# Attention feeding two mixture-of-experts layers: k's leading parts cast on ScalarE one head further ahead, a finished batch's routing and squares spread anew over eight heads

## The chip, the cores and the metric

One core of one Trainium2 chip. The metric is the device time of one execution in microseconds, taken as the median of several runs; lower is better.

## What is computed

Three stages, one feeding the next. q, k, v are 4 batches x 8 heads x 576 rows x 64 columns; f is a forget gate per row. The two expert layers have 8 experts each, 512 -> 1024 -> 512, and every token goes to its best expert alone.

```python
scores = scale * q @ k.T + cum[:, None] - cum[None, :]      # cum = cumsum(log f), causal mask
attn = softmax(scores); x = (attn @ v), heads side by side   # 2304 tokens x 512
# layer 1: expert = argmax(cosine of x and expert_emb), gate = its softmax probability (with tau)
# layer 2: expert = argmax(x @ w_gate), gate = its softmax probability
out = gate * relu(x @ w1[expert]) @ w2[expert]
```

All matrix products are kept near fp32: an operand is split into a leading part (a cast to fp32r, a float32 form that TensorE takes) and the rest, and the products of leading x leading, rest x leading and leading x rest are summed.

## The kernel before, in words

Every engine has its own instruction stream, written out by hand in the order in which it runs; the streams meet only through semaphores. There is no planner. A wait at the head of a stream holds back all that stands behind it on that engine.

**Attention** takes the first 270 us or so: a loop over 32 heads (h = 8 b + hh, batch b, place hh) on every engine. In head h TensorE does the transposed scores of head h (`by_key`, five blocks, L407) and, between them, the plain scores of head h+1 (`by_query`, L395), whose row minima serve as the softmax shift. It then does `weighted` (probabilities times v, L426), turns the finished output of head h-1 back (`back`, L437), brings the minima of head h+1 into one row (`minima_row`, L419), and ends with the last three `weighted` blocks. `by_key(h+1, 0)` waits for `row_ready`.

- SyncE (loop at L336) issues the loads. In pass h it loads q and k of head h+2, each twice, once for either half of the partitions (`load_qk`, L289: q, k, q, k), then the cumulative rows, then, after `pv_done >= h` (the weighted sums of head h-1), v of head h+2. In even passes from 16 on it loads a chunk of expert weights (L358). In passes 6, 10, 14, ... it stores half a batch of finished rows (`store_rows`, L361 to L363).
- ScalarE (L711): `keep_ot(h-1)` copies the output sums out of PSUM, `exps(h, 0..4)` take the exponentials, `leading_q(h+2)` (L661) casts q after the third of them, and `row_in(h+1)` (L675) at the end brings the row of minima into the operand and raises `row_ready`. Between `exps(h, 4)` and `row_in` stand, in batches 1 to 3, the squares of the rows of the finished batch (`g_square`, L685, five per batch), the exponential of its logits (`route_exp`, L691), and, in the eight odd heads from 17 on (SPLIT_AT), the cast of a weight chunk (`split_hi`, L700).
- VectorE (L1127): `leading_k(h+2)` (L823, the cast of k, 128 x 576), one `routing_step` of the finished batch (L1104), the masked minima of head h+1 (`mins`, L861, five blocks) with `rest_k(h+2)` (L837) between, `rest_q(h+2)` (L830), `norm(h-1)` (L903), which waits for `back`, and `split_lo` (L1086) in the SPLIT_AT heads.
- GpSimd (L1344): `copy_k(h+2)` (L1289) copies the cast k for a second operand and stands first in the pass, so behind `leading_k(h+2)`; then `clear(h, 0..4)` (L1294) zero the masked triangle of each exponential block, with `copy_q(h+2)` between. `norms` (L1329) and `scatter` (L1336, table entries of a finished batch by indirect DMA) end the passes named in the diff.

k of head h is held raw in one of two buffers (`k_raw`), its cast in one of three (`kA`). `weighted(h, 0)` waits for `clear(h, 0)`. TensorE waits for all five `mins` before `back` and `minima_row`, and for `rank_read` at hh = 3, `first_read` at hh = 0 and `vals_done` at the end of hh = 7.

**The expert layers** (about 290 to 903 us) are two loops over experts and their tiles of 128 tokens. The change does not touch them.

Of the kernel before, what the change touches and what calls it, by code (L numbers as in the profile page):

```python
# [21 lines left out]
def attention_moe_moe(nc, q_t, k_t, v_p, f, emb_t, tau, w1a, w2a, wg, w1b, w2b, out):  # L22
    B, H, D, S = q_t.shape
    E, DM, FF = w1a.shape
    HEADS = B * H
    TOK = B * S
    NRT = TOK // P
    QT = (S + P - 1) // P
# [26 lines left out]
    with ExitStack() as ctx:  # L55
# [3 lines left out]
        def sem(name):  # L59
            return ctx.enter_context(nc.semaphore(name))  # L60

        def sems(name, n):
            return [sem(f"{name}{i}") for i in range(n)]
# [65 lines left out]
        def asb(name, shape, dt=F32):  # L129
            return attention.enter_context(nc.sbuf_tensor(name, shape, dt))  # L130
# [3 lines left out]
        k_raw = [asb(f"k_raw{a}", [2 * D, S]) for a in range(2)]  # L134
# [3 lines left out]
        kA = [asb(f"kA{a}", [2 * D, SP_], F32R) for a in range(3)]  # L138
# [71 lines left out]
        q_in, k_in, c_in, v_in = sems("q_in", 2), sems("k_in", 2), sems("c_in", 3), sems("v_in", 3)  # L210
        q_hi, k_hi, q_cp, k_cp, q_lo, k_lo = (sem(n) for n in ("q_hi", "k_hi", "q_cp", "k_cp", "q_lo", "k_lo"))
        s_done, t_done = sems("s_done", QT), sems("t_done", QT)
# [444 lines left out]
        def _(act):  # L657
# [3 lines left out]
            def leading_q(h):  # L661

                act.wait_ge(q_in[h % 2], (h // 2 + 1) * 32)
                if h >= 3:
                    act.wait_ge(t_done[QT - 1], h - 2)
                act.mul(qA[h % 3][:], q_raw[h % 2][:], SCALE).then_inc(q_hi, 1)

            def exps(h, t):

                act.wait_ge(t_done[t], h + 1)  # L670
                M = P if t < FT else LR
                act.activation(probT[0:M, PT_AT[t]:PT_AT[t] + S - t * P], ps[0:M, T_AT[t]:T_AT[t] + S - t * P], ACT.Exp,  # L672
                               scale=-1.0).then_inc(exps_done, 1)
# [11 lines left out]
            def g_square(b, t, width=DM):  # L685
                sq = act.activation(squares[:, t, 0:width], o_rows[b % 2][:, t, 0:width], ACT.Square,
                                    accum_out=ssq[:, b * QT + t:b * QT + t + 1])
                if t == QT - 1:
                    sq.then_inc(ssq_done, 1)
# [21 lines left out]
            for h in range(HEADS):  # L711
                b, hh = h // H, h % H
                if h > 0:
                    keep_ot(h - 1)
                exps(h, 0)
                exps(h, 1)
                exps(h, 2)
                if h + 2 < HEADS:
                    leading_q(h + 2)
                exps(h, 3)  # L720
                exps(h, 4)
                if b > 0 and hh == 1:
                    act.wait_ge(norm_done, b * H)
                    g_square(b - 1, 0)
                    g_square(b - 1, 1)
                if b > 0 and hh == 2:
                    g_square(b - 1, 2)
                    g_square(b - 1, 3)
                if b > 0 and hh == 3:
                    g_square(b - 1, 4)  # L730
                if b > 0 and hh == 5:
                    route_exp(b, b - 1)
                if h in SPLIT_AT:
                    split_hi(0, SPLIT_AT.index(h), 1)
                if h + 1 < HEADS:
                    row_in(h + 1)
# [62 lines left out]
        def _(dve):  # L799
# [23 lines left out]
            def leading_k(h):  # L823

                dve.wait_ge(k_in[h % 2], (h // 2 + 1) * 32)
                if h >= 3:
                    dve.wait_ge(t_done[QT - 1], h - 2)
                dve.tensor_copy(kA[h % 3][:, 0:S], k_raw[h % 2][:]).then_inc(k_hi, 1)  # L828

            def rest_q(h):  # L830
# [171 lines left out]
            def place_batch(b):  # L1002

                lo = b * QT
                link(dve.tensor_reduce(rank_f[:, lo:lo + QT], pos[:, lo:lo + QT, :], AX.X, ALU.add),
                     dve.tensor_reduce(ohs[:], oh[:, lo:lo + QT, :].rearrange("p g e -> p e g"), AX.X, ALU.add))
                link(dve.tensor_copy(rank_i[:, lo:lo + QT], rank_f[:, lo:lo + QT]),
                     dve.tensor_tensor(scum[0][:], scum[0][:], ohs[:], ALU.add))
                dve.sem_inc(sum_done, 1)

            def enter_batch(b):

                lo = b * QT
                ent = entry0[:, lo:lo + QT, :]
                link(dve.tensor_scalar(rtile_i[:, lo:lo + QT], rank_i[:, lo:lo + QT], 7, None, ALU.arith_shift_right))
                link(dve.scalar_tensor_tensor(out=part_f[:, lo:lo + QT], in0=rtile_i[:, lo:lo + QT], scalar=1.0 - P * SPP,
                                              in1=region[:, lo:lo + QT], op0=ALU.mult, op1=ALU.add))
                dve.scalar_tensor_tensor(out=ent[:, :, 3], in0=rank_f[:, lo:lo + QT], scalar=float(SPP),
                                         in1=part_f[:, lo:lo + QT], op0=ALU.mult, op1=ALU.add)

            def key_batch(b):

                lo = b * QT
                link(dve.scalar_tensor_tensor(out=key[:], in0=first_i[:, lo:lo + QT], scalar=2.0 * P, in1=rank_f[:, lo:lo + QT],
                                              op0=ALU.mult, op1=ALU.add))
# [78 lines left out]
            def routing_step(b, hh):  # L1104

                if hh == 0 and b > 1:
                    add_firsts(b - 2)
                if hh == 1:
                    largest_batch(b - 1)
                if hh == 2:  # L1110
                    choose_batch(b - 1)
                if hh == 3:
                    read_ranks(b - 1)
                    place_batch(b - 1)
                if hh == 4:
                    key_batch(b - 1)
                    hot_batch(0)
                    hot_batch(1)
                if hh == 5:
                    enter_batch(b - 1)  # L1120
                    scale_batch(b - 1)
                if hh == 6:
                    gate_batch(b - 1)
                if hh == 7:
                    parts_batch(b - 1)

            for h in range(HEADS):  # L1127
                b, hh = h // H, h % H
                n, m = h + 1, h + 2
                if m < HEADS:  # L1130
                    leading_k(m)
                if b > 0:
                    routing_step(b, hh)
                if n < HEADS:
                    mins(n, 4)
                    mins(n, 3)
                if m < HEADS:
                    rest_k(m)
                if n < HEADS:
                    mins(n, 2)  # L1140
                    mins(n, 1)
                    mins(n, 0)
                if m < HEADS:
                    rest_q(m)
                if h == 0:
                    embedding_rows()
                    token_columns()
                else:
                    norm(h - 1)
                if h in SPLIT_AT:  # L1150
                    split_lo(0, SPLIT_AT.index(h), 1)
# [110 lines left out]
        def _(pool):  # L1262
# [73 lines left out]
            def scatter(b, tiles):  # L1336

                pool.wait_ge(ent_done[0], b + 1)
                for t in tiles:
                    pool.indirect_dma_start(out=tab[0], out_offset=bass.IndirectOffsetOnAxis(  # L1340
                        ap=entry0[:, b * QT + t, 3:4], axis=0), in_=entry0[:, b * QT + t, :], in_offset=None,
                        bounds_check=E * TOK - 1, oob_is_err=False).then_inc(g_ent_out, 16)

            for h in range(HEADS):  # L1344
                b, hh = h // H, h % H
                if h + 2 < HEADS:
                    copy_k(h + 2)
                clear(h, 0)
                clear(h, 1)
                clear(h, 2)  # L1350
                if h + 2 < HEADS:
                    copy_q(h + 2)
                clear(h, 3)
                clear(h, 4)
                if b > 0 and hh == 4:
                    norms(b - 1)
                if b == 1 and hh == 6:
                    pool.wait_ge(s_init, 64)
                if b > 0 and hh >= 6:
                    scatter(b - 1, range(hh - 6, hh - 5))  # L1360
                if b > 1 and hh < QT - 2:
                    scatter(b - 2, range(hh + 2, hh + 3))
            scatter(B - 2, range(2, QT))
            norms(B - 1)
            chain = Counter(pool, "pool_chain", pchain[0])

# [127 lines left out]
```

## Time and profile before

| what | us |
|---|---|
| median of 3 runs | 910.94 |
| the three runs | 904.73, 910.94, 911.35 |
| the profiled execution, its own time | 905.14 |
| its span, first to last instruction | 903.6 |

| engine | busy us | share of the span |
|---|---|---|
| TensorE matmuls (PE) | 862.4 | 95% |
| TensorE weight loads (PEld) | 709.3 | 79% |
| VectorE (DVE) | 575.3 | 64% |
| ScalarE (ACT) | 403.8 | 45% |
| GpSimd (POOL) | 293.9 | 33% |

The span is the time between the first and the last instruction; the execution's own time has 1.5 us around it. Busy shares are averages over stages with different limits. The ends of matmuls are modelled, so TensorE may show as busy while it waits briefly. Numbers in the prediction are from the one profiled execution. SPq is SyncE's queue.

### The profile page before, as it was taken

To read this page: it belongs to the slowest core of one execution; us is meant where nothing else is said; L and a number is where in the kernel's file an instruction comes from. 1 tells how busy PE (TensorE), PEld (TensorE's weight loads), DVE (VectorE), ACT (ScalarE), POOL (GpSimd) and SP (SyncE) were. 2 spreads that over 40 slices of the span, in tenths; PEclk is the share of its full clock that TensorE was granted. 3 is DMA by queue.
4 is the path that set the end of the run, shared out by engine and by line. 5 is a ranking of instruction groups with operands and counts; after the bars stand their busy time and mean duration, and the time that the engine had idled before them with its cause. 6 is when DMAs were issued, how large, how long until landed. Compare 5 with 4: busy or idle time off the path is not lost.

```text
span 903.6 us, 16352 instructions
## 1 busy us (share of the span) xinstructions
PE 862.4 (95%) x5025; PEld 709.3 (79%) x5026; DVE 575.3 (64%) x1723; ACT 403.8 (45%) x708; POOL 293.9 (33%) x459
## 2 busy tenths in 40 slices
PE   6999999999997899999999999969999999999995
PEld 5788777777776788888888888858888888888884
DVE  7777888888876576757487767536652264425643
ACT  2455645646652553535265535205551254324541
POOL 7344455345435422233133222222122121122120
PEclk7999999999999999999999999989999999999998
DMA  4334444544522854334265544306652162516100
GB/s 133 95 103 128 128 123 131 152 141 126 169 63 72 296 172 170 124 129 160 98 206 172 169 156 136 113 26 227 217 187 95 35 226 69 189 41 223 46 26 23
DMA packets 59244, 119.63 MB, mean 132 GB/s; under 512 B 11934, under 2 KB 20638, under 8 KB 59204
## 3 DMA queue, kind: packets, MB, share of 16 engines
q1 hardware_dynamic: 49620, 96.93, 33.2%
q0 software_dynamic: 9440, 22.18, 7.5%
q8 instruction: 19, 0.31, 0.1%
q14 instruction: 21, 0.17, 0.1%
q10 hardware_dynamic: 144, 0.04, 0.0%
HBM read 104.13 MB, written 17.99 MB: 135 GB/s over the span
## 4 chain that ended last, share of the span: by engine, by line
PE 80%; DVE 11%; DMA 3%; issue 3%; SPq 1%; POOL 1%; ACT 0%; POOLq 0%; DVEq 0%; ACTq 0%
PE ps L636 27%; PE ps L607 26%; PE ps L445 8%; PE ps L432 5%; PE ps L440 4%; DVE ps L868 3%; PE ps L450 2%; PE ps L403 2%; PE ps L415 2%; PE ps L416 1%; PE ps L404 1%; DVE kA L840 1%; DMA k_raw<-in_k 1%; DVE kA L828 1%; DVE hot L1029 1%
## 5 line engine op out<-in xcount | busy, mean ns | idle before, releaser
L1089 DVE TENSOR_TENSOR wlo<-stage,whi 128x1024 fp32r<-128x1024 f32 x136 | 160.0, 1221 | 31.8 <-ACT whi L703 30.3
L703 ACT CAST whi<-stage 128x1024 fp32r<-128x1024 f32 x136 | 133.6, 1057 | 0.0
L768 ACT ACTIVATE h_s<-ps 128x512 f32<-128x512 f32 x44 | 26.3, 598 | 219.9 <-PE ps L607 219.9
L432 PE MATMUL ps<-probT,v_s 128*65 128x448 f32 (+4 forms) x384 | 103.3, 391 | 3.5 <-POOL probT L1299 3.4
L636 PE MATMUL ps<-whi,hT_hi 128*128 128x512 f32 x352 | 99.5, 404 | 0.0
L636 PE MATMUL ps<-whi,hT_lo 128*128 128x512 f32 x352 | 99.1, 403 | 0.0
L607 PE MATMUL ps<-whi,xT_hi 128*128 128x512 f32 x352 | 94.9, 392 | 3.0 <-DVE xT_lo L1195 3.0
L607 PE MATMUL ps<-whi,xT_lo 128*128 128x512 f32 x352 | 95.2, 392 | 0.0
L636 PE MATMUL ps<-wlo,hT_hi 128*128 128x512 f32 x352 | 95.0, 392 | 0.0
L607 PE MATMUL ps<-wlo,xT_hi 128*128 128x512 f32 x352 | 94.9, 392 | 0.0
L868 DVE CUSTOM_DVE_ANT_0 ps<-ps,maskf 128x576 f32<-128x576 f32 (+4 forms) x160 | 75.3, 510 | 20.6 <-PE ps L404 19.2
L672 ACT ACTIVATE probT<-ps 128x576 f32<-128x576 f32 (+4 forms) x160 | 66.2, 435 | 41.8 <-PE ps L416 38.1
L607 PEld LDWEIGHTS ps<-whi,xT_hi 128*128 128x128 f32 x352 | 65.7, 188 | 18.2 <-ACT xT_hi L759 3.5
L636 PEld LDWEIGHTS ps<-wlo,hT_hi 128*128 128x128 f32 x352 | 66.2, 188 | 14.7
L607 PEld LDWEIGHTS ps<-wlo,xT_hi 128*128 128x128 f32 x352 | 66.1, 188 | 14.7
L607 PEld LDWEIGHTS ps<-whi,xT_lo 128*128 128x128 f32 x352 | 66.2, 188 | 14.2
L1227 DVE TENSOR_TENSOR hT_lo<-ps,hT_hi 128x512 fp32r<-128x512 f32 x44 | 30.4, 690 | 71.4 <-ACT hT_hi L775 71.2
L636 PEld LDWEIGHTS ps<-whi,hT_lo 128*128 128x128 f32 x352 | 63.0, 189 | 11.2
L636 PEld LDWEIGHTS ps<-whi,hT_hi 128*128 128x128 f32 x352 | 62.8, 188 | 11.1
L415 PE MATMUL ps<-qB,kB 97*128 97x288 f32 (+2 forms) x192 | 69.5, 371 | 0.3 <-ACT probT L672 0.3
L1371 POOL COPY ent_next<-ent_tab 128x4 int32 (+1 forms) x45 | 8.6, 192 | 182.8 <-DVE ent_mid L1196 181.5
L1243 DVE COPY y_idx<-ent_cur 128x1 int32<-128x1 int32 x44 | 6.7, 152 | 94.2 <-PE ps L636 94.2
(223 smaller groups left out, 1626.6 us busy)
## 6 DMA issues: line engine op xcount, KB each, us to landing
stage<-in_moe_w SPq DMA_DIRECT2D x128, 512.0 KB, 4.3
q_raw<-in_q SPq DMA_DIRECT2D x64, 144.0 KB, 3.0
k_raw<-in_k SPq DMA_DIRECT2D x64, 144.0 KB, 3.1
v_s<-in_v SPq DMA_DIRECT2D x32, 162.5 KB, 2.3
x<-o_rows SPq DMA_DIRECT2D x8, 512.0 KB, 3.9
kB<-cum_hl SPq DMA_DIRECT2D x64, 2.2 KB, 1.7
table<-entry POOLq DMA_INDIRECT x44, 2.5
table<-tinit SPq DMA_DIRECT2D x2, 288.0 KB
```

Source lines behind the costliest of these rows:

```text
L415: pe.matmul(o, kB[a][0:ROW + 1, k0:k0 + P], qB[a][0:ROW + 1, lo:hi], start=True, stop=False)
L432: mm = pe.matmul(ps[0:D + 1, OT_AT + lo:OT_AT + hi], v_s[h % 3][:, t, :], probT[:, col:col + hi - lo], start=(t == 0), stop=(t == QT - 1 o ...
L440: mm = pe.matmul(back_ps[:, t, :], o_t[:, t * P:(t + 1) * P], i_emb[:, h % H, :], start=True, stop=True)
L445: mm = pe.transpose(bank[:, c * P:(c + 1) * P], src[:, c * P:(c + 1) * P], ident[:])
L607: mm = pe.matmul(h_ps[hf], x[:, c * P:(c + 1) * P], w1_sl(w[b], c, hf * 512, 512), start=(wi == 0 and c == 0), stop=(wi == 2 and c == DC - 1))
L636: mm = pe.matmul(y_ps, h[:, kk * P:(kk + 1) * P], w2_sl(w[b], kk), start=(hf == 0 and wi == 0 and kk == 0), stop=(hf == 1 and wi == 2 and ...
L672: act.activation(probT[0:M, PT_AT[t]:PT_AT[t] + S - t * P], ps[0:M, T_AT[t]:T_AT[t] + S - t * P], ACT.Exp, scale=-1.0).then_inc(exps_done, 1)
L703: act.copy(whi[b][:, c, :], stage[:, c, :]).then_inc(w_hi[c], 1)
L768: act.activation(h_s[:, 0:512], h_ps[0], ACT.Relu).then_inc(h_relu[0], 1)
L868: dve.tensor_tensor_reduce(out=tile, in0=tile, in1=maskf[0:M, at:at + q1], scale=1.0, scalar=LARGE, op0=ALU.add, op1=ALU.min, accum_out=sm ...
L1089: dve.tensor_tensor(wlo[b][:, c, :], stage[:, c, :], whi[b][:, c, :].bitcast(F32), ALU.subtract).then_inc(w_lo[c], 1)
L1227: dve.tensor_tensor(hT_lo[:, 0:512], hT_ps[0], hT_hi[:, 0:512].bitcast(F32), ALU.subtract).then_inc(h_lo[0], 1)
```

## The change

- `leading_k` for heads 2 and up moves from VectorE to ScalarE. ScalarE does it for head h+3 after `exps(h, 4)`, ahead of the squares, the weight cast and `row_in`; in head 0 also for head 2, between `leading_q(2)` and `exps(0, 3)`. VectorE keeps heads 0 and 1. The new one waits for `k_in`, both halves of k of head h+3.
- The squares of a finished batch are spread as 1, 2, 1, 1 over hh = 1 to 4 (before 2, 2, 1 over hh = 1 to 3); its `route_exp` moves from hh = 5 to 6.
- On VectorE: `key_batch` from hh = 4 to 3, `enter_batch` from 5 to 4, the two `hot_batch` from 4 to 5, `scale_batch` from 5 to 6, `gate_batch` from 6 to 7; `parts_batch` stays in 7.
- On GpSimd the scatters of a batch move by one head: tile 0 in hh = 7, tiles 1 to 4 in hh = 0 to 3 of the batch after, and for batch 2 its tiles 1 to 4 after the loop (before: tiles 0 and 1 in hh = 6 and 7, tiles 2 to 4 in hh = 0 to 2, or after the loop).

```diff
+            def leading_k(h):
+
+                act.wait_ge(k_hi, h)
+                act.wait_ge(k_in[h % 2], (h // 2 + 1) * 32)
+                act.copy(kA[h % 3][:, 0:S], k_raw[h % 2][:]).then_inc(k_hi, 1)
...
                 if h + 2 < HEADS:
                     leading_q(h + 2)
+                if h == 0:
+                    leading_k(2)
                 exps(h, 3)
                 exps(h, 4)
+                if h + 3 < HEADS:
+                    leading_k(h + 3)
                 if b > 0 and hh == 1:
                     act.wait_ge(norm_done, b * H)
                     g_square(b - 1, 0)
+                if b > 0 and hh == 2:
                     g_square(b - 1, 1)
-                if b > 0 and hh == 2:
                     g_square(b - 1, 2)
+                if b > 0 and hh == 3:
                     g_square(b - 1, 3)
-                if b > 0 and hh == 3:
+                if b > 0 and hh == 4:
                     g_square(b - 1, 4)
-                if b > 0 and hh == 5:
+                if b > 0 and hh == 6:
                     route_exp(b, b - 1)
...
             def leading_k(h):
 
                 dve.wait_ge(k_in[h % 2], (h // 2 + 1) * 32)
-                if h >= 3:
-                    dve.wait_ge(t_done[QT - 1], h - 2)
                 dve.tensor_copy(kA[h % 3][:, 0:S], k_raw[h % 2][:]).then_inc(k_hi, 1)
...
                 if hh == 3:
                     read_ranks(b - 1)
                     place_batch(b - 1)
+                    key_batch(b - 1)
                 if hh == 4:
-                    key_batch(b - 1)
+                    enter_batch(b - 1)
+                if hh == 5:
                     hot_batch(0)
                     hot_batch(1)
-                if hh == 5:
-                    enter_batch(b - 1)
+                if hh == 6:
                     scale_batch(b - 1)
-                if hh == 6:
+                if hh == 7:
                     gate_batch(b - 1)
-                if hh == 7:
                     parts_batch(b - 1)
...
-                if m < HEADS:
-                    leading_k(m)
...
-                if b == 1 and hh == 6:
+                if b == 1 and hh == 7:
                     pool.wait_ge(s_init, 64)
-                if b > 0 and hh >= 6:
-                    scatter(b - 1, range(hh - 6, hh - 5))
-                if b > 1 and hh < QT - 2:
-                    scatter(b - 2, range(hh + 2, hh + 3))
-            scatter(B - 2, range(2, QT))
+                if b > 0 and hh == 7:
+                    scatter(b - 1, range(1))
+                if b > 1 and hh < QT - 1:
+                    scatter(b - 2, range(hh + 1, hh + 2))
+            scatter(B - 2, range(1, QT))
             norms(B - 1)
```

## Rows read from the trace of the kernel before

**Rows 1.** Who waited for whom, 20 to 270 us: total us, times, longest us
```profile
POOL kB L1292 <- DVE kA L828: 94.5, 29, 5.0
ACT qB L678 <- PE ps L422: 62.5, 31, 2.8
...
PEld ps L440 <- DVE smin L868: 21.9, 30, 1.0
```

**Rows 2.** Timeline of ScalarE, head 3: start us, length us, instruction, [idle before]
```profile
43.95 0.63 ACT L678 CAST qB<-ps 1x576 fp32r<-1x576 f32 x1 [2.39 <-PE ps L422]
...
48.42 0.67 ACT L672 ACTIVATE probT<-ps 128x192 f32<-128x192 f32 x2 [0.58 <-PE ps L416]
51.48 0.63 ACT L678 CAST qB<-ps 1x576 fp32r<-1x576 f32 x1 [2.39 <-PE ps L422]
```

**Rows 3.** Timeline of all engines, heads 16 and 17
```profile
150.41 1.19 PEld L440 LDWEIGHTS ps<-i_emb,o_t 65*128 65x128 f32 x10 [0.54 <-DVE smin L868]
...
153.07 0.46 DVE L828 CAST kA<-k_raw 128x576 fp32r<-128x576 f32 x1
...
153.60 0.66 POOL L1292 CAST kB<-kA 64x576 fp32r<-64x576 f32 x1 [1.58 <-DVE kA L828]
...
153.66 0.65 DVE L973 TENSOR_TENSOR eqi<-lg_raw,mx 128x40 f32<-128x40 f32 x1
...
154.34 0.20 DVE L974 SCALAR_TENSOR_TENSOR eqi<-eqi,iota 128x40 f32<-128x40 f32 x1
```

**Rows 4.** Timeline of ScalarE: the row of minima entering heads 9 and 29
```profile
89.19 0.63 ACT L678 CAST qB<-ps 1x576 fp32r<-1x576 f32 x1 [2.39 <-PE ps L422]
...
252.00 0.63 ACT L678 CAST qB<-ps 1x576 fp32r<-1x576 f32 x1 [2.84 <-PE ps L422]
```

**Rows 5.** Timeline of SyncE's DMA issues, loads of head 6; then the last one's landing
```profile
44.92 0.33 SPq L301 DMA_DIRECT2D v_s<-in_v  x1
...
47.24 0.60 SPq L293 DMA_DIRECT2D k_raw<-in_k  x1
...
DMA to landing us min/median/max: 2.9/2.9/2.9
```

**Rows 6.** The same issues for head 21's loads; then the last one's landing
```profile
160.90 0.34 SPq L301 DMA_DIRECT2D v_s<-in_v  x1
...
163.25 1.25 SPq L292 DMA_DIRECT2D q_raw<-in_q  x1
...
165.89 0.60 SPq L293 DMA_DIRECT2D k_raw<-in_k  x1
...
DMA to landing us min/median/max: 4.0/4.0/4.0
```

**Rows 7.** Timeline of ScalarE, end of head 17
```profile
157.71 0.61 ACT L686 ACTIVATE squares<-o_rows 128x512 f32<-128x512 f32 x1
...
158.32 1.03 ACT L703 CAST whi<-stage 128x1024 fp32r<-128x1024 f32 x1
159.93 0.63 ACT L678 CAST qB<-ps 1x576 fp32r<-1x576 f32 x1 [0.57 <-PE ps L422]
```

**Rows 8.** Timeline of head 0: ScalarE's third exponential block and q cast, TensorE's first weighted sum
```profile
24.75 0.44 ACT L672 ACTIVATE probT<-ps 128x320 f32<-128x320 f32 x1 [0.22 <-PE ps L416]
25.08 0.68 ACT L666 ACTIVATE qA<-q_raw 128x576 fp32r<-128x576 f32 x1
...
24.97 1.13 PE L432 MATMUL ps<-probT,v_s 128*65 128x128 f32 x4
```

**Rows 9.** Timeline at the tail: TensorE after a wait, GpSimd's norms
```profile
288.54 0.41 PE L474 MATMUL ps<-vals,hot 128*128 128x3 bf16 x10 [2.68 <-DVEq L1041]
...
281.34 1.20 POOL L1333 TENSOR_TENSOR nrm<-ssq,half 128x5 f32<-128x5 f32 x1 [3.12 <-DVEq L1162]
```

**Rows 10.** Engines in stretches of 4 us: stretch, its length, busy us per engine, granted clock, DMA
```profile
284.00:288.00 4.00, 1.86 (x37) 1.68 (x33) 3.09 (x16) 0.24 (x1) 1.59 (x1) 1.00 0.00 0
288.00:292.00 4.00, 3.12 (x37) 3.04 (x38) 2.92 (x20) 0.00 (x0) 3.06 (x4) 0.67 0.53 157
```

## The prediction

> **What bounds the kernel now.** I read the totals by engine first, then who waited for whom in the attention loop, then the timelines of single heads, last SyncE's issues with their landings. The change touches attention alone, so the rest of the span counts only as a shift.
>
> A plain head shows the pace: the row of minima enters at 43.95 and again at 51.48 [rows 2], 7.53 us later. TensorE has no idle time there, so 7.53 is its own work. From head 9 to head 29 the same row moves from 89.19 to 252.00 [rows 4]: 20 heads in 162.8, where 20 plain ones take 150.6. Of the 12.2 more, about 1.9 is TensorE's own: three rank products and two sets of first slots, about 0.4 each by the slots' row [rows 9]. The remaining 10.3 is waiting, and the waits name VectorE: TensorE's weight loads for `back` sit 21.9 us behind the minima [rows 1], of which 0.54 in each head belong to the plain pace. With 0.4 outside these 20 heads I put VectorE's share at 10.7.
>
> Why VectorE is late in batches 1 to 3: its chain norm, k cast, routing step, minima has no gap. The cast costs 0.46, and GpSimd's copy of k starts right after it, 153.60 to 154.26; the routing op that starts at 153.66 takes 0.65 where its neighbour of the same shape takes 0.20 [rows 3]. So the cast brings a stall of 0.45 behind it. The Trainium skill, "SBUF — State Buffer", on the shared port pair, says that a VectorE op with two SBUF inputs and a GpSimd op that reads SBUF exclude each other for the whole instruction; the trace agrees with its 0.65.
>
> **The change part by part.**
>
> *VectorE loses the cast and the stall behind it*, 0.9 a head, and the steps are spread so that neither `hot_batch` nor a weight split stacks as before. The largest excesses, 1.9 in heads 19 and 27, had both. After removal I work out chains of 6.5 to 7.6 against a pace of 7.53. Gain: the 10.7, less 0.3 that may stay. In head 1 a late `copy_k` held TensorE too; I count 0.5 there.
>
> *Head 0.* `copy_k(2)` stands first in GpSimd's pass, ahead of `clear(0, 0)`, and TensorE's first weighted sum waits for that clear. Before, k of head 2 was cast long ahead. Now ScalarE casts it behind `leading_q(2)`, which runs from 25.08 to 25.76 [rows 8]; one cast of 128 x 576 follows by 0.60 to 0.68, then the copy 0.66 [rows 3], then a clear of some 0.25: 27.3, where the weighted sum started at 24.97 [rows 8]. Loss 2.3, with nothing to cover it.
>
> *The cast on ScalarE.* By itself it is hidden: between the last exponential, ending at 49.09, and the row at 51.48 ScalarE idles 2.39 [rows 2] and the cast takes 0.68 at most. With a square (0.61) and a weight split (1.03) [rows 7] it is 2.3, which just fits.
>
> *The wait it brings is not hidden.* In head c ScalarE now needs k of head c+3. SyncE cannot issue that load before the weighted sums of head c-1 are over. In a plain head v is issued at 44.92, the fourth of q, k, q, k at 47.24, and it lands 2.9 later at 50.1 [rows 5]: 6.2 after the row of minima entered, with 7.53 allowed. The cast needs 0.65 with the wake-up, ending at 6.9: it fits by 0.6. VectorE before used the same k a head later, so these landings cost nothing. Now `row_in` stands behind the cast on ScalarE, and all of TensorE behind `row_in`.
>
> The margin is gone where something stands ahead of the load in SyncE's queue. For head 21 a weight chunk and two row stores precede: v is issued at 160.90, the first q at 163.25, the last k at 165.89, landing 4.0 later at 169.9 [rows 6]. The row entered head 18 at 159.93 [rows 7], so the offset is 9.96. Cast 0.65 and two squares 1.24 bring 11.85, against 7.53: 4.3 late. The rank products behind `weighted` cover 0.35 and a carry from head 17 about 0.2: 3.8.
>
> The same subtraction over the 28 heads gives an offset of 6.1 to 6.9 in most, harmless or nearly so, and these: head 6 7.7, 10 7.6, 12 7.8, 14 8.3, 16 8.2, 18 10.0, 20 7.4, 22 9.4, 24 7.9, 26 9.4, 28 7.6. With the work queued behind each cast, and with this correction: a delayed `row_in` does not delay the weighted sums ahead of it, so the next load starts on time and the next head has that much more room. Late by 0.8, 1.6, 1.5, 1.6, 1.0, 3.8, 1.1, 2.75, 0.7, 3.1, 1.3; heads 17 and 25, with square and split, 0.6 together; the other fifteen 0.05 each. Sum 20.6. Bounds: nothing, if ScalarE never waits, and 29, the same without the correction.
>
> *Clock.* TensorE then stands still for 3 to 4 us a few times. After a wait of 2.68 that ended at 288.54 [rows 9] the granted clock of 288 to 292 is 0.67 where it was 1.00 [rows 10], that is, part of it at 1.2 GHz: 1.3 us of work lost. With four such waits (heads 0, 18, 22, 26), even chances each, I take 2, bounds 0 and 6. The Trainium skill, "TensorE: Matmul & The Clock Gate", section "HAM oscillation — how this bites in real kernels", warns that kernels which wait for loads between bursts of matmuls fall back to the lower clock; it speaks against this change, and rows 10 bear it out for one wait.
>
> *The rest.* Squares in hh = 4 make GpSimd's norms, 1.20 [rows 9], end nearer to the next clear; about 0.4 of room stays. At the end one scatter more precedes the last norms, which had 3.12 idle before them [rows 9]; a scatter takes about 1.3 with its issue. Hidden: 0. Without cover it would cost those 1.3. Bounds of both together -0.5 to 1.5.
>
> Sum against the profiled execution: 905.1 - 10.7 + 0.3 - 0.5 + 2.3 + 20.6 + 2 = 919.1. That execution is 5.8 below the median of 910.94, while one run of the three (904.73) lies beside it. I put the forecast between 919.1 and 924.9, in the middle: 922.
>
> **The rivals.**
>
> *The loads are in time after all (faster).* If the landings come before ScalarE gets there, for instance because SyncE runs ahead, only the gain stays: 905.1 - 10.7 - 0.5 + 2.3 = 896. For it: ScalarE's 2.39 of idle time in a plain head. Against it: the 6.9 of the plain head leave only 0.6, and rows 6 show landings that nobody waited for before. It decides from an offset of about 6.9 on: if the late heads stay under that, it is faster.
>
> *Half the lateness.* If queue and landing shrink in the late heads, as where the 4.0 and more of a landing was chance, the sum of 20.6 becomes 10 and the two sides nearly cancel: 905.1 - 11 + 2.3 + 10 = 906 to 912 on the scale of the median.
>
> *The clock falls in most stalls, and casts come so late that GpSimd's copy meets VectorE's norm.* Every stall above 2 us costs 1.3 to 2 and the copy 0.45 in VectorE-bound heads: 919.1 + 6 + 4 = 929. For it: rows 10. Against it: 284 to 288, with TensorE busy for 1.86 of 4 us, still had 1.00 [rows 10].
>
> *The change doesn't relieve VectorE,* since the copy of k only moves from the routing step to the norm: 8 of the 10.7 stay, 922 + 5 = 927, with the 3 that fall where ScalarE decides anyway left out. Against it: the norm reads PSUM in most of its ops.
>
> **How the numbers follow.** Forecast 0.50, own range 915 to 928; all loads in time 0.10; half the lateness 0.22; clock and copies 0.12; no relief 0.06. Forecast 922, range for 8 in 10: 904 to 931. A measurement here tells about 1% from no change. Faster by over 1%: the first rival and a little of the second, 0.13. Within 1%: most of the second and the forecast's lower edge, 0.25. Slower: 0.62.
>
> **What the profile after would show.** ScalarE's casts of k with idle time before them that ends with the landing of k, longest in heads 18, 22 and 26 (near 4, 3 and 3 us) and next to none in odd heads. TensorE waiting for the row of minima from ScalarE, about 20 in sum over the loop, where it waited for VectorE's minima; VectorE with clear idle time before its minima; the first weighted sum near 27.3. Heads at 7.53 between the late ones. If instead ScalarE's idle time still stands before `row_in` and ends with TensorE, the loads are in time and I am wrong; if the late heads are there but under 1 us each, only the size is off.

## The result, and the profile after

The changed kernel takes 925.98 us (median of 4, 922.35 to 928.28) against 910.15 for the kernel before: ratio 1.0185, 95% interval 1.0149 to 1.0221. It is slower by nearly two per cent. Its profiled execution took 925.05, with a span of 923.0 where that of before was 903.6.

From the page of the changed kernel: busy time by engine, and the chain that ended last, by line.

```profile
PE 868.5 (94%) x5025; PEld 717.5 (78%) x5026; DVE 558.5 (61%) x1693; ACT 424.2 (46%) x738; POOL 298.1 (32%) x459
...
PE ps L636 27%; PE ps L607 26%; PE ps L445 8%; PE ps L432 7%; DMA k_raw<-in_k 4%; PE ps L440 3%; PE ps L415 2%; PE ps L403 2%; PE ps L416 2%; PE ps L404 2%; PE ps L450 2%; SPq L292 2%; PE ps L481 1%; ACT kA L672 1%; SPq L293 1%
```

TensorE's busy time has grown by 6 us although its instructions are the same 5025: part of its work ran at a lower clock. And "DMA k_raw" stands in the chain with 4%: for some 37 us of the span the chain runs through a load of k.

Who waited for whom, as in [rows 1], here from 20 to 290 us, since the loop is longer:

```profile
DVE ps L877 <- PE ps L404: 49.2, 45, 5.3
ACT kA L672 <- DMA k_raw<-in_k: 45.3, 22, 4.5
...
POOL kB L1299 <- ACT kA L672: 38.8, 21, 4.5
...
PEld ps L440 <- DVE smin L877: 17.2, 30, 0.9
PEld ps L415 <- ACT qB L684: 16.9, 11, 3.6
...
ACT qB L684 <- PE ps L422: 13.2, 14, 2.3
```

The list has turned round. GpSimd waited 94.5 for the cast of k and waits 38.8. The wait of `row_in` for TensorE, 62.5 before, is 13.2. In its place ScalarE's cast of k waits 45.3 for the load, 22 times and up to 4.5, and TensorE's first key product waits 16.9 for the row of minima from ScalarE, 11 times. VectorE waits 49.2 for products where it had 18 before: it is relieved, and nobody profits.

ScalarE at the end of head 18, the counterpart of [rows 2] and [rows 7]:

```profile
166.90 0.63 ACT L684 CAST qB<-ps 1x576 fp32r<-1x576 f32 x1
...
171.32 0.68 ACT L678 ACTIVATE probT<-ps 128x192 f32<-128x192 f32 x2 [0.58 <-PE ps L416]
176.49 0.67 ACT L672 CAST kA<-k_raw 128x576 fp32r<-128x576 f32 x1 [4.50 <-DMA k_raw<-in_k]
177.07 0.62 ACT L692 ACTIVATE squares<-o_rows 128x512 f32<-128x512 f32 x1
...
178.41 0.63 ACT L684 CAST qB<-ps 1x576 fp32r<-1x576 f32 x1
```

The last exponentials end at 172.00. The cast waits 4.50 for k, then come the two squares, and the row of minima enters at 178.41, 11.5 after the one before it; the plain pace is 7.53. SyncE's issues for that k, the counterpart of [rows 6]:

```profile
167.60 0.34 SPq L301 DMA_DIRECT2D v_s<-in_v  x1
...
169.92 1.38 SPq L292 DMA_DIRECT2D q_raw<-in_q  x1
...
172.62 0.60 SPq L293 DMA_DIRECT2D k_raw<-in_k  x1
```

With 3.8 from the last issue to the landing, k is there at 176.4.

The heads by length in us, from the first key product of one head to that of the next. TensorE's own work is 7.53, in heads 10, 18, 26 with the rank products 7.88, in 15 and 23 with the first slots 7.95:

| head | 0 | 1 | 6 | 10 | 11 | 12 | 14 | 16 | 18 | 19 | 20 | 22 | 23 | 25 | 26 | 27 | 28 |
|---|---|---|---|---|---|---|---|---|---|---|---|---|---|---|---|---|---|
| before | 6.86 | 8.08 | 7.54 | 7.88 | 7.53 | 8.29 | 7.53 | 7.53 | 8.74 | 7.88 | 9.44 | 8.45 | 8.35 | 7.88 | 8.75 | 7.52 | 9.44 |
| after | 8.92 | 7.54 | 8.23 | 9.53 | 9.09 | 8.38 | 9.00 | 8.43 | 11.52 | 8.96 | 8.97 | 10.13 | 9.62 | 8.42 | 10.62 | 10.47 | 9.24 |

All 31 heads together take 263.7 where they took 246.0. Head 0 of the kernel before ran in part at the lower clock (granted 0.61 from 20 to 24 us); in spread_only, where it did not, it took 6.41.

### The profile page after: what moved, and what is told of

The parts are those of the page before. It is cut to its first block, busy times and chain, and to the rows that moved or that the text cites. A ratio compares the mean times of both kernels' runs of the same rounds, so it can differ in the third digit from the quotient of the medians.

```text
span 923.0 us, 16371 instructions
## 1 busy us (share of the span) xinstructions
PE 868.5 (94%) x5025; PEld 717.5 (78%) x5026; DVE 558.5 (61%) x1693; ACT 424.2 (46%) x738; POOL 298.1 (32%) x459
## 4 chain that ended last, share of the span: by engine, by line
PE 82%; DMA 6%; SPq 4%; ACT 3%; issue 2%; DVE 2%; POOL 1%; POOLq 0%; DVEq 0%; ACTq 0%
PE ps L636 27%; PE ps L607 26%; PE ps L445 8%; PE ps L432 7%; DMA k_raw<-in_k 4%; PE ps L440 3%; PE ps L415 2%; PE ps L403 2%; PE ps L416 2%; PE ps L404 2%; PE ps L450 2%; SPq L292 2%; PE ps L481 1%; ACT kA L672 1%; SPq L293 1%
## 5 line engine op out<-in xcount | busy, mean ns | idle before, releaser
L432 PE MATMUL ps<-probT,v_s 128*65 128x448 f32 (+4 forms) x384 | 105.9, 400 | 2.3 <-POOL probT L1306 2.3
L415 PE MATMUL ps<-qB,kB 97*128 97x288 f32 (+2 forms) x192 | 72.1, 384 | 15.8 <-ACT qB L684 15.5
L1306 POOL TENSOR_SCALAR_AFFINE_SELECT probT<-probT 128x128 f32<-128x128 f32 (+1 forms) x160 | 44.5, 286 | 90.6 <-ACT probT L678 86.0
L636 PEld LDWEIGHTS ps<-whi,hT_lo 128*128 128x128 f32 x352 | 63.0, 189 | 11.5
L636 PEld LDWEIGHTS ps<-whi,hT_hi 128*128 128x128 f32 x352 | 62.9, 189 | 10.9
```

Of the source, the lines that this page charges most:

```text
L415: pe.matmul(o, kB[a][0:ROW + 1, k0:k0 + P], qB[a][0:ROW + 1, lo:hi], start=True, stop=False)
L432: mm = pe.matmul(ps[0:D + 1, OT_AT + lo:OT_AT + hi], v_s[h % 3][:, t, :], probT[:, col:col + hi - lo], start=(t == 0), stop=(t == QT - 1 o ...
L636: mm = pe.matmul(y_ps, h[:, kk * P:(kk + 1) * P], w2_sl(w[b], kk), start=(hf == 0 and wi == 0 and kk == 0), stop=(hf == 1 and wi == 2 and ...
L1306: pool.affine_select(out=block, in_=block, compare_op=ALU.is_ge, fill=0.0, base=0, pattern=[[1, M]], channel_multiplier=-1).then_inc(clear ...
```

## The experiments

Ratios are to the kernel before, timed on the same chip beside each kernel. "Loop" is the same 31 heads in the profiled execution (before 246.0, changed 263.7).

**spread_only.** ScalarE's `leading_k` and its calls are taken out, VectorE's put back as before; all else is the changed kernel.

```diff
-                if h + 3 < HEADS:
-                    leading_k(h + 3)
...
+                if m < HEADS:
+                    leading_k(m)
                 if b > 0:
                     routing_step(b, hh)
```

> Half the change: squares, routing steps and scatters spread anew, the cast of k left on VectorE one head later. Theory (the loss is ScalarE's wait for k ahead of the row of minima): no such wait here, so no loss; heads 19 and 27 lose one stacked hot step (1 us each), heads 12, 20 and 28 gain 0.4 each: 1 to 3 us faster than the kernel before. Rival (the new spread itself delays ScalarE, GpSimd's norms or TensorE): 8 to 20 us slower.

Measured: ratio 0.9991 (0.9973 to 1.0008), loop 244.8. The spread alone is harmless and gains 1.2 us of loop, too little to show in the time.

**cast_only.** The other half, on the kernel before: ScalarE casts k as in the change, VectorE's cast is taken out.

```diff
                 exps(h, 4)
+                if h + 3 < HEADS:
+                    leading_k(h + 3)
                 if b > 0 and hh == 1:
                     act.wait_ge(norm_done, b * H)
                     g_square(b - 1, 0)
```

> The other half: the cast of k on ScalarE one head further ahead, with squares, routing steps and scatters as before. Theory: the whole loss is here, 13 to 21 us slower than the kernel before, with ScalarE idle until k has landed for 40 to 50 us in sum. Rival (spread): within 1% of before or faster, since VectorE is relieved.

Measured: ratio 1.0146 (1.0116 to 1.0176), loop 259.7. Its waits:

```profile
ACT kA L672 <- DMA k_raw<-in_k: 44.2, 21, 3.9
...
PEld ps L415 <- ACT qB L684: 16.2, 12, 3.0
```

The loss is in the cast's new place, with the same two waits as in the changed kernel.

**k_first.** The changed kernel, with SyncE's four loads of a head in another order.

```diff
-                for side in range(2):
-                    sp.dma_start(q_raw[a][side * D:(side + 1) * D, :], q_h[h]).then_inc(q_in[a], 16)
-                    sp.dma_start(k_raw[a][side * D:(side + 1) * D, :], k_h[h]).then_inc(k_in[a], 16)
+                order = ("q", "k", "q", "k") if h < 4 else ("k", "k", "q", "q")
+                for n, what in enumerate(order):
+                    side = n % 2 if h >= 4 else n // 2
+                    raw, src, done = (q_raw, q_h, q_in) if what == "q" else (k_raw, k_h, k_in)
+                    sp.dma_start(raw[a][side * D:(side + 1) * D, :], src[h]).then_inc(done[a], 16)
```

> The changed kernel with SyncE issuing k, k, q, q from head 4 on in place of q, k, q, k: the second half of k is issued 1.28 us earlier. Theory: the lateness of 19.4 us over the heads falls to about 8 to 9, and the lower clock shows after one to three heads instead of four: 12 to 16 us faster than the changed kernel, 908 to 914. Rival (ScalarE is slow because it has one more cast per head, not because it waits): no difference, 923 to 928.

Measured: ratio 1.0052 (1.0035 to 1.0068), so 12 us faster than the changed kernel (1.0185 - 1.0052 of 911), loop 249.9. Of the wait for k this is left:

```profile
ACT kA L674 <- DMA k_raw<-in_k: 19.9, 10, 4.1
```

19.9 for 45.3, with ScalarE's own work unchanged. That rules out the rival of an overloaded ScalarE: moving one issue by 1.28 us takes most of the loss away.

**queue.** The changed kernel, in which SyncE issues weight chunks and row stores ahead of its wait for the weighted sums.

```diff
                     load_c(h + 2)
+                    others()              # the weight chunk and the stores of pass h
                     if h > 0:
                         sp.wait_ge(pv_done, h)
                     load_v(h + 2)
```

> The changed kernel with SyncE's weight chunks and row stores issued before it waits for the weighted sums, so that nothing but v stands between that wait and the loads of q and k. Theory: landing offsets of heads 6, 10, 14, 18, 22, 26 fall from 7.5 to 9.5 us to 6.2 to 6.5, those of 16, 20, 24, 28 by some 0.5; lateness about 7 in sum and none above 1.6, so no lower clock: 16 to 20 us faster than the changed kernel, 904 to 910. Rival (not SyncE's queue but the landing time under load sets the offset): offsets fall by less than 1 and the time stays above 918.

Measured: ratio 1.0054 (1.0035 to 1.0073), loop 252.3: 12 us faster than the changed kernel, not 16 to 20. Heads 10, 18, 22 and 26 fell from 9.5, 11.5, 10.1, 10.6 to 8.3, 8.3, 7.6 and 9.5, and no head from 10 on ran at the lower clock. What I had missed is head 19: the last k issue, then ScalarE's cast, square and weight cast:

```profile
177.21 0.71 SPq L293 DMA_DIRECT2D k_raw<-in_k  x1
...
181.89 0.67 ACT L677 CAST kA<-k_raw 128x576 fp32r<-128x576 f32 x1 [2.02 <-DMA k_raw<-in_k]
182.47 0.63 ACT L697 ACTIVATE squares<-o_rows 128x512 f32<-128x512 f32 x1
...
183.09 1.03 ACT L714 CAST whi<-stage 128x1024 fp32r<-128x1024 f32 x1
```

That k took 4.6 from issue to landing, with a 512 KB weight chunk issued behind it at 180.86; head 19 is 9.37 long. Both halves of the offset count, the queue and the landing. Heads 21, 25 and 26, at 8.7, 8.9 and 9.5, are late too. Head 0 cost 11.6 here, at the lower clock; more on that below.

**behind_row.** The changed kernel, with the cast of head h+3 behind `row_in(h+1)`.

```diff
-                if h + 3 < HEADS:
-                    leading_k(h + 3)
...
                 if h + 1 < HEADS:
                     row_in(h + 1)
+                if h + 3 < HEADS:
+                    leading_k(h + 3)
```

> The changed kernel with ScalarE's cast of k for head h+3 placed behind row_in(h+1) in place of ahead of exps' followers, so that the wait for k no longer holds the row of minima. Theory: heads whose k lands 6.2 to 7.5 us after the row lose nothing; only those over about 8.5 still hold the copy of the output and the first exponentials: lateness 19.4 falls to 5 to 8, at most one stretch of lower clock: 10 to 17 us faster than the changed kernel (ratio to before 1.000 to 1.008). Rival (one more cast per head on ScalarE is what costs): the cast now stands directly ahead of the exponentials, so no gain or worse, ratio 1.018 or more.

Measured: ratio 1.0043 (1.0014 to 1.0072), loop 249.5: 13 us faster than the changed kernel. ScalarE in a plain head:

```profile
60.47 0.63 ACT L684 CAST qB<-ps 1x576 fp32r<-1x576 f32 x1 [2.39 <-PE ps L422]
61.12 0.67 ACT L672 CAST kA<-k_raw 128x576 fp32r<-128x576 f32 x1
61.70 0.63 ACT L689 COPY o_t<-ps 65x576 f32<-65x576 f32 x1
62.23 1.07 ACT L678 ACTIVATE probT<-ps 128x576 f32<-128x576 f32 x2
```

Here the cast waits for k only 4 times, 4.0 us in all, and its own 0.6 us shows: the plain heads 3 to 9 take 7.71 for 7.53. Taken for all 29 heads, these 0.18 make an estimate of 5 us for the cast's work ahead of the exponentials, against the 19 and more that its wait costs ahead of the row. Head 19 alone, 10.96 long, was still at the lower clock.

**fill.** The changed kernel with small matmuls in four of TensorE's waits.

```diff
+                if h in FILL:             # {11: 24, 19: 44, 23: 36, 27: 40}
+                    pe.wait_ge(exps_done, QT * h)
+                    for _ in range(FILL[h]):
+                        pe.matmul(ps[:, T_AT[0]:T_AT[0] + P], identb[:], onesb[:], start=True, stop=True)
                 pe.wait_ge(row_ready, h + 1)
```

> The changed kernel with 24, 44, 36 and 40 small bf16 matmuls on TensorE in its waits ahead of heads 11, 19, 23 and 27, into a region that the next product overwrites. Every wait for k stays as it is. Theory (7.6 of the loss is TensorE's lower clock after those waits): heads 11, 19, 23 and 27 fall from 9.1, 9.0, 9.6 and 10.5 us to 7.6 to 8.1, 5 to 7 us faster than the changed kernel, ratio 1.011 to 1.013. Rival (those heads are long because their k or exponentials are late): they stay at 9 and more, ratio 1.0185.

Measured: ratio 1.0167 (1.0135 to 1.0199), which cannot be told from the changed kernel's. In the profile heads 11, 19, 23 and 27 fell from 9.09, 8.96, 9.62, 10.47 to 7.54, 7.55, 7.99, 7.55: 7.5 us, as the theory has it. TensorE ahead of head 19:

```profile
177.56 2.62 PE L505 MATMUL ps<-onesb,identb 128*128 128x128 bf16 x44
180.97 0.40 PE L416 MATMUL ps<-qB,kB 97*128 97x288 f32 x1 [0.79 <-ACT qB L689]
...
181.62 0.37 PE L416 MATMUL ps<-qB,kB 97*128 97x448 f32 x1
```

The wait is still there, filled for 2.62 of its length, and the product of 448 columns behind it takes 0.37 where the changed kernel's takes 0.57. By its time it is a miss: 1.011 to 1.013 was expected. In the profiled execution, at 929.50 the slowest of the four, the 7.5 us are outweighed by 3.5 more in head 0 (12.4 for 8.9), 1.7 in the four heads ahead of the fills, and 7.4 behind the loop, 4.6 of them before the first expert product. The other three, 926.3 to 927.5, have no profile, so what held them up is not shown. Head 0 in this kernel, and the same stretch in the changed one (columns as in [rows 10]):

```profile
28.00:32.00 4.00, 4.00 (x14) 2.91 (x13) 1.08 (x6) 1.11 (x3) 1.74 (x6) 0.50 0.00 0
```

```profile
28.00:32.00 4.00, 4.00 (x30) 3.13 (x29) 3.10 (x13) 2.50 (x6) 1.55 (x4) 1.00 0.01 1
```

Up to that point both programs are alike and both TensorEs waited 2.3 us, though fill's products ahead of the wait had already lost 0.5 to the lower clock. After the wait the clock stood at 0.50 in the first, the 1.2 GHz level, and at 1.00 in the other.

**head2.** The changed kernel, with k of head 2 cast on VectorE at the start of pass 0.

```diff
+                if h == 0:
+                    leading_k(2)          # VectorE
```

> The changed kernel with k of head 2 cast on VectorE at the start of pass 0, as before; ScalarE starts with head 3. Theory: head 0 falls from 8.92 to 6.9 us and nothing else moves: 2.1 us faster than the changed kernel, ratio 1.016. Rival (GpSimd's first clear waits for something else): head 0 stays.

Measured: ratio 1.0220 (1.0177 to 1.0263), a miss by its time. Head 0 fell from 8.92 to 7.49, still with part of its products at the lower clock; but heads 19, 23 and 27 took 10.2, 10.9 and 10.4 for 9.0, 9.6 and 10.5, by a longer low clock, and the loop is 263.0. So head 0 gave back 1.4 of the 2.1 expected, with a granted clock of 0.83, and the loop is 0.7 shorter. The time is longer by what lies behind the loop, which took 9 us more than in the changed kernel's profile: 4.7 before the first expert product, and 4.3 in the expert layers, where the granted clock from 600 to 645 us was 0.81 for 0.92.

**with_q.** ScalarE casts k of head h+2 right behind `leading_q(h+2)`, when it has long landed.

```diff
                     leading_q(h + 2)
+                    leading_k(h + 2)                        # ScalarE, no cast of h + 3
...
-                if h + 2 < HEADS:
-                    copy_k(h + 2)
                 clear(h, 0)
                 clear(h, 1)
                 clear(h, 2)
                 if h + 2 < HEADS:
                     copy_q(h + 2)
+                    copy_k(h + 2)                           # GpSimd
...
-                if m < HEADS:
-                    rest_k(m)
                 if n < HEADS:
                     mins(n, 2)
                     mins(n, 1)
                     mins(n, 0)
                 if m < HEADS:
+                    rest_k(m)                               # VectorE
                     rest_q(m)
```

> The changed kernel with ScalarE's cast of k for head h+2, not h+3, right behind leading_q(h+2); GpSimd's copy of k moves behind its copy of q, and VectorE's rest_k behind the last of the minima. Theory: VectorE keeps its relief and the k it needs landed a head ago, so nobody waits for a load: all heads at 7.5 to 7.9 us, loop 8 to 10 us shorter than in the kernel before, ratio 0.989 to 0.993. Rival (ScalarE or GpSimd becomes the bound with the cast and copy between the exponentials): heads of 8 us and more throughout, ratio 1.01 or above.

Measured: 903.70 against 911.14, ratio 0.9912 (0.9884 to 0.9941), loop 234.9: faster than both kernels. `row_in`, with its first and last start, in this kernel, in the changed one and in the one before:

```profile
L684 ACT CAST qB<-ps x32: 626/626/627, 18.6 to 256.3; 1x576 fp32r<-1x576 f32 x32
```

```profile
L684 ACT CAST qB<-ps x32: 626/626/627, 18.6 to 285.1; 1x576 fp32r<-1x576 f32 x32
```

```profile
L678 ACT CAST qB<-ps x32: 626/626/627, 18.6 to 267.4; 1x576 fp32r<-1x576 f32 x32
```

The last row of minima enters 11.1 earlier than before. No head is over 7.6 but for TensorE's own additions.

**copy_late.** Of with_q only the moves of GpSimd's copy and of `rest_k`, on the kernel before; VectorE keeps the cast and the routing stays.

> The kernel before with two moves only: GpSimd's copy of k behind its copy of q, and VectorE's rest_k behind the last of the minima. VectorE keeps the cast of k, and routing is spread as before. If VectorE's lateness of 10.7 us was mainly the stall behind GpSimd's copy (0.45 in a routing step, and rest_k held by the copy of q), heads with one light step fall to 7.53 and some 5 to 7 us go, ratio 0.992 to 0.995. Rival (the cast itself, 0.46 a head, is the larger share): under 3 us, ratio 0.997 or above.

Measured: 903.46 against 912.65, ratio 0.9903 (0.9885 to 0.9922), a little more than expected, loop 237.8. VectorE's `rest_k` and the routing op of [rows 3] in heads 9 to 30:

```profile
L840 DVE TENSOR_TENSOR kA<-k_raw,kB 64x576 fp32r<-64x576 f32 x22 | 16.4, 746 | 0.0
...
L973 DVE TENSOR_TENSOR eqi<-lg_raw,mx 128x40 f32<-128x40 f32 x3 | 0.6, 200 | 0.1
```

The routing op takes 0.20 in each batch. So 8.2 of the 11.1 us of loop that with_q gains come without moving the cast off VectorE at all. The stall is not the only thing that goes with the copy, though. In the kernel before, the copy stood ahead of GpSimd's clears and waited for VectorE's late cast, and TensorE waited for the clear:

```profile
PE ps L432 <- POOL probT L1299: 3.4, 6, 1.1
```

In copy_late this row is gone, so up to 3.4 of the 8.2 may be this second path. No run parts it from the stall, or from the move of `rest_k`; and since seven heads were late by 0.35 only, taking away either the stall or the cast's 0.46 may be enough there. What stays is 0.6 in head 19, 1.1 to 1.2 in heads 20 and 28, where hot steps and weight splits meet, and 0.2 to 0.4 in heads 22 and 23.

**with_q_old.** with_q with routing, squares and scatters as in the kernel before.

> with_q (cast of k on ScalarE right behind leading_q of the same head, copy and rest_k late) with squares, routing and scatters as in the kernel before. Theory: only heads 20 and 28, where two hot steps and a weight split meet, stay over 7.53, by about 1 us each, so 2 us slower than with_q, ratio 0.991 to 0.994. Rival (the new spread carries most of with_q's gain): ratio above 0.995.

Measured: 903.18 against 912.65, ratio 0.9894 (0.9872 to 0.9916), just under the range expected, loop 235.8: with the copy already moved, taking the cast off VectorE is worth 2.0 more. Heads 20 and 28 stay over by 0.7 each, 1 us in sum more than with_q, which the time does not resolve: the intervals of the last three overlap.

## Why the prediction was right, and where a size was off

The forecast was 922, range 904 to 931, slower; it is 925.98. The sum itself was 919.1 for the profiled execution, which took 925.05; that the forecast lies nearer owes something to the 2.9 put on for the median.

**VectorE's relief, -10.7.** Right in size: with head 0, the wait and the clock taken off, 11.4 is left. Heads 13, 17, 21 and 24, over by 0.2 to 0.35 before, are at 7.54 to 7.74 or held by ScalarE. The routing op stalled behind the copy takes less too:

```profile
L982 DVE TENSOR_TENSOR eqi<-lg_raw,mx 128x40 f32<-128x40 f32 x3 | 0.9, 297 | 0.1
```

0.30 on average for 0.64. Three readings behind the term were off. The row that it names, 21.9, holds only 5.7 beyond the 0.54 of each of 30 heads; another 3.4 is the wait for GpSimd's clear shown under copy_late, so the late cast also held TensorE through GpSimd. The largest excesses, 1.9, are in heads 20 and 28 (9.44 each), not 19 and 27. And it gave cast and stall equal weight, where moving the copy alone gained 8.2 (`rest_k` too takes 0.75 on average there, 0.86 before) and the cast on top 2.0.

**Head 0, +2.3.** Right: the cast on ScalarE, the copy, the clear and TensorE's first weighted sum, as reckoned one after the other:

```profile
24.55 0.68 ACT L666 ACTIVATE qA<-q_raw 128x576 fp32r<-128x576 f32 x1
...
25.12 0.66 ACT L672 CAST kA<-k_raw 128x576 fp32r<-128x576 f32 x1
...
25.85 0.65 POOL L1299 CAST kB<-kA 64x576 fp32r<-64x576 f32 x1 [3.89 <-ACT kA L672]
26.47 1.29 POOL L1306 TENSOR_SCALAR_AFFINE_SELECT probT<-probT 128x128 f32<-128x128 f32 x3
...
26.90 1.16 PE L432 MATMUL ps<-probT,v_s 128*65 128x128 f32 x4 [2.31 <-POOL probT L1306]
```

TensorE waited 2.31; the head is 2.06 longer than before and 2.5 longer than the 6.41 of spread_only.

**The wait for k, 20.6.** Right in kind and size. Over TensorE's own pace the heads held by ScalarE are longer by 19.4 in sum: head 18 by 3.6 (3.8 forecast), 26 by 2.7 (3.1), 22 by 2.6 (2.75), 10 by 1.65 (1.6), 14 by 1.5 (1.6), 28 by 1.7 (1.3), 20 by 1.4 (1.1), 12 by 0.85 (1.5), where the long landing of before, 4.5, did not come again (3.8). cast_only, k_first and behind_row each show the cause: the place of the cast, the landing of k, and what stands behind the wait. Also right is the correction: a late row doesn't hold the next load, and so heads 11, 13, 15 and 21 have time to spare.

**The clock, +2.** This is the term that was mis-sized: 7.6. That is above the bound of 6 that it gave. The prediction priced the lower clock from one stretch at 1.3 us, gave it even chances, and counted on heads 0, 18, 22 and 26; head 0's wait cost nothing in clock, and head 10's did. Heads 10 and 18, each with the wait at its end, and the heads 11, 19, 23 and 27 that follow a long wait (columns as in [rows 10]):

```profile
99.86:109.39 9.53, 8.04 (x59) 6.40 (x58) 6.48 (x28) 5.84 (x14) 3.19 (x7) 1.00 0.54 159
109.39:118.48 9.09, 9.09 (x51) 7.17 (x52) 5.56 (x16) 5.06 (x11) 2.71 (x7) 0.81 0.23 66
167.57:179.09 11.52, 8.06 (x58) 6.41 (x58) 7.53 (x28) 5.84 (x14) 4.72 (x8) 1.00 0.76 215
179.09:188.05 8.96, 8.96 (x52) 7.52 (x52) 4.80 (x16) 6.10 (x12) 4.66 (x8) 0.81 0.08 23
...
214.69:224.31 9.62, 9.62 (x61) 7.48 (x62) 6.55 (x24) 5.59 (x11) 4.32 (x8) 0.82 0.22 63
...
251.02:261.49 10.47, 10.47 (x51) 8.43 (x52) 5.13 (x16) 6.11 (x12) 4.26 (x8) 0.69 0.13 38
```

Each of the four heads behind a long wait has a mean clock of 0.69 to 0.82, and is 1.4 to 2.9 longer than its own work. How it looks in the products: the first at 179.09 comes after 3.46 of waiting, and the 448-column product takes 0.57 and 0.37 within one head.

```profile
179.09 0.61 PE L415 MATMUL ps<-qB,kB 97*128 97x288 f32 x1 [3.46 <-ACT qB L684]
...
180.22 0.57 PE L415 MATMUL ps<-qB,kB 97*128 97x448 f32 x1
...
182.65 0.37 PE L404 MATMUL ps<-kA,qA 128*128 128x448 f32 x1
```

The Trainium skill, "TensorE: Matmul & The Clock Gate", section "HAM oscillation — how this bites in real kernels", says that waits between bursts bring the lower clock back. The trace agrees for four waits, of 1.49, 3.46, 2.06 and 2.56, with 0.69 to 0.82 in the heads behind them, and not for head 0's 2.31. fill shows that the idle time is the cause, since with the same wait filled the four heads are back at their pace. It is one execution, and for head 11 it decides little, as that head kept its clock in head2 and cast_only without a fill; heads 19 and 27 lost theirs in both of these. The third rival had the clock fall in most stalls: it was nearer to the truth in that than the forecast. Its other half, and the fourth rival, had VectorE's `norm` held by the copy in its new place; the norm's two main ops take 491 and 189 ns on average in both kernels.

**The rest.** Squares, norms and scatters cost nothing, as spread_only shows. Up to the first expert product 1.2 us were lost (granted clock over that stretch 0.88 for 0.94), and 0.5 in the expert layers. In sum: loop 17.7 for the 14.0 of the forecast. The difference of 3.7 is 5.6 more from the clock, less 1.2 in the wait for k, 0.5 by more relief of VectorE, and 0.2 in head 0.

## What to carry to other kernels

Before an operation goes one step further ahead, read when its input lands, not only how long it takes: a landing that nobody waited for stands in no wait of the profile, and the new place may be in front of what sets the pace. Put a cast behind the wait that its engine has anyway, and where its data are a step old. When VectorE's ops take 0.65 in one place and 0.20 in another, look first at what GpSimd starts beside them; here moving that copy and `rest_k` gained 8.2 us of loop, and moving the work on top of it 2.0. The work in a harmless place, with the copy left where it was, was not tried. A time that doesn't follow the edit asks for a look at the stretches that the edit doesn't touch: in fill and head2 they differ by 7 and 9 us.

## What the runs showed that was not expected

A wait of about the same length does not always bring the clock down. In k_first it fell behind heads 18 and 22, after waits of 1.72 and 1.93, and not behind head 26, after 1.74. In changed, cast_only and head2 the lower clock followed all eight waits of 2.06 and more at the ends of heads 18, 22 and 26. Head 0, with the same wait of 2.3 us, took 8.9 in the profiles of changed, cast_only, k_first and behind_row, and 12.4 in fill and 11.6 in queue.

Between the loop and the first expert product the profiled kernels took 28.0 (before) and 29.2 (changed), and 33 to 36 in all others, faster or slower. In k_first TensorE's warm-up matmuls there came in pieces, with idle time that ended with nothing the profile shows:

```profile
294.30 4.66 PE L483 MATMUL ps<-onesb,identb 128*128 128x128 bf16 x48 [0.34 <-DVE tiles_i L1191]
300.19 0.27 PE L483 MATMUL ps<-onesb,identb 128*128 128x128 bf16 x2 [1.23 <-issue]
301.61 0.27 PE L483 MATMUL ps<-onesb,identb 128*128 128x128 bf16 x2 [1.15 <-issue]
303.05 0.58 PE L483 MATMUL ps<-onesb,identb 128*128 128x128 bf16 x4 [1.17 <-issue]
```

Such gaps, 0.3 to 1.2 us each, stand in the profiles of all ten experiments and in neither of before and changed, so some 5 us between a profiled experiment and these two are not its edit's. That may be why runs of the kernel before lie at 904.7 and at 909 to 916; what they are is open, and no kernel was made to try it.
